# Four small tiles declared earlier: later tiles of SBUF move by 96 or 128 bytes

## The reference

```python
sig = 1.0 / (1.0 + np.exp(-f_logit))
f = lower_bound + (1.0 - lower_bound) * sig
i = 1.0 - f
for t in range(S):                       # S = 6080
    h = f[:, t] * h + i[:, t] * x[:, t]
    y[:, t] = h
hid = y.reshape(B * S, D) @ w_in         # (12160, 256) @ (256, 2048)
r = np.maximum(hid, 0.0)
out = (r * r) @ w_out                    # (12160, 2048) @ (2048, 256)
```

## Time and profile before

| | before |
|---|---|
| median of the runs | 1053.62 us |
| lowest and highest run | 1053.40 and 1055.32 us |
| the profiled execution's own time | 1053.4 us |
| its span, first to last instruction | 1051.6 us |
| TensorE busy | 1043.5 us (99%) |
| VectorE busy | 590.7 us (56%) |
| ScalarE busy | 525.3 us (50%) |
| mean granted clock of TensorE | 0.998 |

### The profile page before, as it was taken

One profiled execution on the slowest core, in us unless ns is written; L12 is line 12 of the kernel. 1 busy time (PEld: TensorE's weight loads), 2 busy tenths in 40 slices (PEclk: granted clock), 3 DMA queues, 4 the chain that ended last, 5 costly groups with the idle time before them and its releaser, 6 DMA issues.

```text
span 1051.6 us, 13223 instructions
## 1 busy us (share of the span) xinstructions
PE 1043.5 (99%) x4622; PEld 867.6 (83%) x4622; DVE 590.7 (56%) x1067; ACT 525.3 (50%) x873; POOL 1.4 (0%) x6
## 2 busy tenths in 40 slices
PE   8999999999999999999999999999999999999998
PEld 5998888888888888888888888888888888888887
DVE  7765555645546556465564655646556455565533
ACT  5555454454554545455454454554545455454453
POOL 0000000000000000000000000000000000000000
PEclk9999999999999999999999999999999999999999
DMA  7110101101011010010110101101011010100000
GB/s 270 41 58 1 58 21 41 60 0 60 22 38 60 0 60 30 30 60 0 60 42 18 60 7 53 57 3 60 19 40 60 0 60 20 40 20 0 21 20 21
DMA packets 21343, 41.75 MB, mean 40 GB/s; under 512 B 1360, under 2 KB 3152, under 8 KB 21328
## 3 DMA queue, kind: packets, MB, share of 16 engines
q1 hardware_dynamic: 21296, 41.56, 11.4%
q0 software_dynamic: 32, 0.00, 0.0%
HBM read 29.10 MB, written 12.45 MB: 40 GB/s over the span
## 4 chain that ended last, share of the span: by engine, by line
PE 99%; DVE 1%; DMA 0%; issue 0%; ACT 0%; POOL 0%; POOLq 0%
PE out_ps L413 49%; PE hidden_ps L397 49%; PE hidden_ps L380 0%; DMA bound<-lower_bound_t 0%; DVE y L294 0%; DVE neg_input L284 0%; DVE forget L276 0%; DVE y_hi L304 0%; ACT result L225 0%; POOL zeros L363 0%; DVE state L303 0%; DVE middle L352 0%; DVE y_lo L310 0%; DVE slope L351 0%; POOLq L454 0%
## 5 line engine op out<-in xcount | busy, mean ns | idle before, releaser
L244 ACT ACTIVATE relu<-hidden_ps 128x512 f32<-128x512 f32 (+1 forms) x384 | 227.8, 593 | 498.3 <-PE hidden_ps L397 495.3
L336 DVE CAST g_hi<-square 128x512 fp32r<-128x512 f32 (+1 forms) x384 | 162.7, 424 | 436.0 <-ACT square L249 436.0
L413 PE MATMUL out_ps<-g_hi,w_out_hi 128*128 128x512 f32 (+1 forms) x768 | 297.3, 387 | 0.1
L413 PE MATMUL out_ps<-g_lo,w_out_hi 128*128 128x512 f32 (+1 forms) x768 | 297.2, 387 | 0.0
L413 PE MATMUL out_ps<-g_hi,w_out_lo 128*128 128x512 f32 (+1 forms) x768 | 297.2, 387 | 0.0
L397 PE MATMUL hidden_ps<-y_hi,w_in_hi 128*128 128x512 f32 (+1 forms) x762 | 295.3, 388 | 0.0
L397 PE MATMUL hidden_ps<-y_lo,w_in_hi 128*128 128x512 f32 (+1 forms) x762 | 295.2, 387 | 0.0
L397 PE MATMUL hidden_ps<-y_hi,w_in_lo 128*128 128x512 f32 (+1 forms) x762 | 295.1, 387 | 0.0
L338 DVE TENSOR_TENSOR g_lo<-square,g_hi 128x512 fp32r<-128x512 f32 (+1 forms) x384 | 263.8, 687 | 13.2
L249 ACT ACTIVATE square<-relu 128x512 f32<-128x512 f32 (+1 forms) x384 | 241.0, 628 | 14.4 <-DVE g_lo L338 0.5
L413 PEld LDWEIGHTS out_ps<-g_hi,w_out_hi 128*128 128x128 f32 x768 | 144.1, 188 | 29.0 <-issue 0.5
(11 more groups left out here) (24 smaller groups left out, 65.5 us busy)
## 6 DMA issues: line engine op xcount, KB each, us to landing
f_in<-f_logit_t SPq DMA_DIRECT2D x22, 512.0 KB, 4.1
x_in<-x_t SPq DMA_DIRECT2D x22, 512.0 KB, 4.8
out_t<-result SPq DMA_DIRECT2D x21, 512.0 KB, 3.1
w_in_raw<-w_in_t SPq DMA_DIRECT2D x2, 512.0 KB, 8.4
w_out_raw<-w_out_t SPq DMA_DIRECT2D x2, 512.0 KB, 9.1
out_t<-result SPq DMA_DIRECT2D x2, 448.0 KB, 2.9
w_in_raw<-w_in_t SPq DMA_DIRECT2D x1, 640.0 KB, 10.9
w_out_raw<-w_out_t SPq DMA_DIRECT2D x1, 640.0 KB, 11.9
```

Source lines behind the costliest of these rows:

```text
L244: nc.scalar.activation(relu[:, k, 0:n], hidden_ps[:, s % HBANKS, 0:n], ACT.Relu).then_inc(relu_done, 1)
L336: nc.vector.tensor_copy(g_hi[:, slot, 0:n], square[:, k, 0:n]).then_inc(g_hi_done, 1)
L413: mm = nc.tensor.matmul(out_ps[:, b, c, 0:n], w[:, j, c * P:(c + 1) * P], v[:, r % GSLOTS, 0:n], start=(j == 0 and w is w_out_hi and v is ...
```

## The change

Four declarations of small tiles are moved up. `bound`, `slope` and `middle` now come ahead of `gate`, and `state` comes ahead of `y`. Nothing else is altered: all engines get the same instructions in the same order with the same waits. All line numbers grow by 22, since blank lines stand at the head of the new file.

```diff
         w_out_hi = sb("w_out_hi", [P, STEPS, C * P], F32R)
         w_out_lo = sb("w_out_lo", [P, STEPS, C * P], F32R)
+        bound = sb("bound", [P, C])
+        slope = sb("slope", [P, C])
+        middle = sb("middle", [P, C])
         gate = sb("gate", [P, C, N])
         forget = sb("forget", [P, C, N])
         neg_input = sb("neg_input", [P, C, N])
+        state = sb("state", [P, B, C])
         y = sb("y", [P, B, C, N])
         y_hi = sb("y_hi", [P, B, C, N], F32R)
         y_lo = sb("y_lo", [P, B, C, N], F32R)
@@
         result = sb("result", [P, B, C, N])
         zeros = sb("zeros", [P, 512], mybir.dt.bfloat16)
-        bound = sb("bound", [P, C])
-        slope = sb("slope", [P, C])
-        middle = sb("middle", [P, C])
-        state = sb("state", [P, B, C])
```

## The result

The changed kernel took 1077.87 us, median of four runs (1077.05 to 1078.28), against 1053.59 for the kernel before in the same comparison. The ratio is 1.0225, with a 95% interval from 1.021 to 1.024: 24.3 us slower, where I had forecast no change. Nothing but addresses differs.

A forecast was written before the change was run, and what follows sets the result against it. TensorE's matmul pace bounds the kernel: an opening of 15.9 us, matmuls at 0.2025 or 0.2267 us each, a tail of 3.2 us. All change terms were 0, giving 1053.6 us against the median, range 1052.0 to 1055.5.

The forecast's parts named there:

- Moving operands of TensorE: `y_hi`, `y_lo`, `g_hi`, `g_lo`, read by all 4608 matmuls, start 128 bytes later: taken as 0, bounds -138 to +41 us.
- rival A: Every matmul slower because moving and weight streams meet in SBUF: 9 ns each, +41 us, 1095 us; chance 0.04.
- Rival B: Every matmul faster, the shared remainder having held the pace up: to 916 us, a tenth giving 1040; chance 0.04.
- TensorE is not held up by others' reads: TensorE's SBUF reads don't wait on other engines': a matmul starts every 0.2267 us in busy and quiet stretches.
- The gate tiles, +96 bytes: 0: `gate`, `forget`, `neg_input`, at 32 by 64: hidden in the loop, uncovered in the opening; taken as 0, at most +0.26 us.
- Rival C: VectorE's part of the opening longer: +0.26 us, 1053.9 us, or 1055.4 with a second low-clock stretch; chance 0.03.
- `bound`, `slope`, `middle`, `state`: Small tiles moved ahead, remainders by 64 unchanged, read as one value per partition: 0.
- `result`: Stores from `result`, +128 bytes, only the last on the path: 0 from rows, at most -0.12 us by the page's rule.
- The clock in the opening: TensorE's lower clock from 13.4 to 16.6 us cost 1.5 us; its scatter, independent of addresses, set the range.

The follow-up runs named there:

- e8: Changed kernel with 128 unused bytes more ahead of `y`, so all tiles from `y` on are at +256; 1053.72 us.
- e3: Kernel before with 128 unused bytes ahead of `w_in_raw` and 128 more ahead of `gate`: weights move by +128, moving operands by +256; 1077.45 us.
- e4: Kernel before with 128 unused bytes ahead of `w_in_raw` alone: weights and moving operands both move by +128; 1053.52 us.
- e13: Kernel before with `w_in_lo` and `w_out_lo` alone moved by 128 by 256, other weights and moving tiles keeping their remainder; 1071.15 us.
- e2: Kernel before with 96 unused bytes ahead of `gate` and 160 ahead of `y`: gate tiles at +96, all from `y` on at +256; 1053.65 us.
- e1: Kernel before with 128 unused bytes ahead of `gate`, so `gate` and all tiles after it move by +128; 1078.03 us.
- e10: Changed kernel with the weight loads of the middle passes (`y_lo`, `g_lo`) halved to 64 columns, writing 64 partitions; 1064.10 us.
- e11: Kernel before with 128 unused bytes ahead of `g_hi` alone: `g_hi` and `g_lo` at distance 128 to the weights; 1071.00 us.
- e6: Kernel before with unused bytes ahead of `y` and `g_hi`: `y` tiles at +96, `g` tiles at +160, weights unmoved; 1082.53 us, one run.
- u32: Kernel before with 32 unused bytes ahead of `y`: all moving operands at distance 32 to the weights; 1080.91 us, two runs.
- u64: Kernel before with 64 unused bytes ahead of `y`: all moving operands at distance 64 to the weights; 1062.42 us, two runs.
- u192: Kernel before with 192 unused bytes ahead of `y`: all moving operands at distance 192 to the weights; 1080.95 us, two runs.
- e12: Kernel before with slot pitch N + 64, `y_hi` and `y_lo` data starting 16 bytes and `g_hi` and `g_lo` 8 bytes into their slots; 1079.42 us.
- e5: Kernel before with unused bytes ahead of `y` and `g_hi`: `y` tiles at +32, `g` tiles at +64, weights unmoved; 1074.90 us, one run.
- e7: Kernel before with unused bytes ahead of `y` and `g_hi`: `y` tiles at +192, `g` tiles at +224, weights unmoved; 1074.18 us, one run.
- e9: Kernel before with the weight loads of the middle passes (`y_lo`, `g_lo`) halved to 64 columns, writing 64 partitions; 1067.12 us.

## Why the prediction was wrong

**The step that failed** is the first group of the change part, "*Moving operands of TensorE ... +128 bytes.* ... I take 0". It was the only term that is multiplied by the number of matmuls; it measured 232.38 - 226.67 = 5.7 ns in the wide ones, 24.1 us in all. The narrow ones add 1.3 ns each, 0.5 us, in these two traces, but by e8 and e3 they vary by more than that at one distance. It was rival A that came true, in its place and under its condition ("with the moving tiles at 0 and the weights at 128 by 256"). Of its mechanism, e3, e4 and e13 show that it takes both streams, the moving operand and the weight load beside it; that they "meet in some part of SBUF" stays an assumption. Its price of 9 ns a matmul was too high by more than half. It was taken from two VectorE instructions that have nothing to do with the case, so that it came within a factor of two is luck. Its chance of 0.04 was far too low.

**Why I took 0.** I leaned on the pace being equal for first and second products and in busy and quiet stretches. The first half of that evidence was empty: all of those tiles stood at distance 0, which the prediction itself says ("the trace has no row with such an operand at another remainder"). A thing that a trace doesn't vary can't be read from it. I should have taken the term as open within its bounds, -138 to +41 us, and left rivals A and B a share of the chance to match.

**TensorE is not held up by others' reads** was right as far as it went. The loss is as large in the quiet end, 24 matmuls in 5.60 us. What the sentence missed is that TensorE reads twice at a time: its own weight loads run beside the matmuls for 83% of the span.

**The gate tiles, +96 bytes: 0.** Right, and shown twice (e2 and the opening's rows above). Rival C had no part.

**`bound`, `slope`, `middle`, `state`: 0.** Right; e8 keeps them moved and takes 1053.72 us.

**`result`.** The last store lands 2.0 us after its issue, where it was 2.1:

```profile
out_t<-result SPq DMA_DIRECT2D x2, 256.0 KB, 2.0
```

It reads 2.0 in all five traces in which `result` starts at 0 by 256 (the changed kernel, e1, e4, e10, e11), and 2.1 in all thirteen others. By the trace's whole ns the last store takes 2014 to 2037 in the five and 2078 to 2110 in the thirteen; the stores of 512 KB, beside TensorE, take 3.05 or 3.06 us in the median against 3.12 or 3.13. So my 0 was wrong here by some 0.08 us. The estimate of at most 0.12 us from the Trainium skill's rule on descriptors ("DMA: Bandwidth & Descriptors", How a descriptor splits into AXI transactions) has the sign and about the size. But counted in beats, remainder 32 (e6) would cost a quarter of what remainder 128 does, and it costs the same: 3.13 and 3.12 us for 512 KB. In no run was `result` moved alone.

**The clock in the opening.** The granted clock of 0.50 falls from 13.4 to 16.6 us before and already holds from 9.0 to 13.4 in the changed kernel:

```profile
9.00:11.50 2.50, 2.40 (x6) 1.82 (x6) 2.43 (x4) 1.04 (x2) 0.00 (x0) 0.50 1.02 365
11.50:13.40 1.90, 1.15 (x4) 0.89 (x4) 1.83 (x5) 0.74 (x2) 0.00 (x0) 0.50 1.04 396
13.40:16.60 3.20, 3.20 (x12) 2.89 (x11) 2.50 (x3) 0.30 (x1) 0.00 (x0) 0.62 1.05 408
16.60:20.00 3.40, 2.60 (x14) 2.10 (x13) 2.45 (x5) 3.34 (x7) 0.00 (x0) 1.00 1.03 403
```

Where it falls differs from run to run (e4 has 0.81, 0.50, 0.50 and 0.88 in these four stretches at 1053.5 us), so this is part of the scatter of some 2 us, and no part of the 24. The prediction gave all of that scatter to the clock, and that isn't shown: in e8 the first matmul of a second product starts 0.8 us earlier than in the kernel before, and the execution is still 0.7 us longer, with narrow matmuls that cost 1.4 us more. The range had been built on this scatter, which is why it was too narrow.

**Rival B** had the right question, whether the shared remainder matters, and the wrong sign for the wide matmuls: in the mean none of the distances tried brought back anything of the 13.3 ns above 512 columns at 2.4 GHz. For the 366 narrow ones its sign came true at distances 32 and 64, by 2.4 and 2.7 ns or 1 us in all, in one trace of each.

## What to carry to other kernels

Where matmuls with float32 (F32R) operands follow each other without a gap, every tile that TensorE reads belongs in the sum, by its address too: look at where the moving tiles start against the weights, by 256 bytes, and keep that remainder when small tiles are declared ahead of them (here 128 bytes of padding won back all 24 us). With another number of columns, measure a few distances: at 448 columns the two best traces are those at 32 and 64 bytes. Read the pace in ns from start to start, and suspect the place of the operands when an even pace turns into a repeating series. A term that multiplies thousands of instructions and that the trace doesn't vary is not 0 but unknown, and a range has to hold its bounds.

## What the runs showed that I had not expected

With float32 operands (F32R) of 512 columns, moving the weights alone (e3) takes a matmul from 226.7 to 232.4 ns, and moving the `_lo` weights alone (e13) slows only the matmul beside the load and the next one. The Trainium skill's page "TensorE: Matmul & The Clock Gate" (Part 2, Step-by-step) says that TensorE has two independent read ports and that loading the next tile's weights doesn't take read bandwidth from the running matmul. These runs disagree with the second statement, and the measurement decides: what a matmul costs depends on where the weights loaded beside it lie. Of the ports themselves they show nothing.

| distance by 256, all moving tiles alike | pace, 512 columns, ns | pace, 448 columns, ns | time, us |
|---|---|---|---|
| 0 (before, e2, e4, e8) | 226.67 | 202.7 (e8 206.5) | 1053.5 to 1053.7 |
| 32 (u32) | 233.33 | 200.3 | 1080.9 |
| 64 (u64) | 228.89 | 200.0 | 1062.4 |
| 128 (after, e1, e3) | 232.38 | 203.9 (e3 206.6) | 1077.5 to 1078.0 |
| 192 (u192) | 233.33 | 202.3 | 1081.0 |

In each row the time follows from the pace of the wide matmuls to within 0.8 us: 4224 x (pace - 226.67) added to 1053.6 gives 1081.7, 1063.0, 1077.7 and 1081.7 us. Shown for 512 columns is that the distance counts and the two places don't, that 256 bytes more change nothing while 128 do, that the load takes part, and that an effect reaches further than the matmul beside the load. Not shown is how the reads collide inside SBUF, why 226.67 ns is where they settle at distance 0, and why a half-length load upsets that. Nor is a distance always one pace: e10 and e12 each took two different times, 19 and 9 us apart, with the same addresses and the same granted clock, so the points with one or two runs (e5 to e7, u32 to u192) may have a second time that wasn't met. A story in which each loaded byte costs a fixed time fell with e9, and I have no other that gives all five paces. Whether other types than this one behave alike wasn't tried. No version beat the kernel before; e2, e4 and e8 equal it.
